# The a and b products of a bilinear layer, taken as seven products of quarters instead of eight

## The chip, the core and the metric

The kernel runs on one core of one Trainium2 chip. The time is that of one execution on the device in microseconds. Before the change it is 843.13 us, the median of 3 runs (842.65 to 844.28). TensorE (PE) multiplies, VectorE (DVE) and ScalarE (ACT) work on tiles in SBUF and in PSUM, GpSimd (POOL) works on SBUF only, and SyncE (SP) issues most transfers.

## The reference, cut to what matters

Attention with decay (4 batches, 8 heads, 576 positions, head size 64) gives x of 2304 tokens by 512. A mixture of 8 experts sends each token through one expert. The last layer takes the result x:

```python
def _moe2_ref(x, w_a, w_b, w_out):
    a = x @ w_a          # 2304x512 @ 512x1536
    b = x @ w_b          # 2304x512 @ 512x1536
    return (a * b @ w_out).astype(np.float32)   # 2304x1536 @ 1536x512
```

All of it is float32.

## The kernel before, in words

Every large product is made of three: an operand v is split into hi, which is v rounded to the fp32r type that PE takes, and lo = v - hi, and PE sums hi*hi, hi*lo and lo*hi in PSUM. So each operand needs a rounding copy and a subtraction somewhere.

The program has three stages on one core: attention with the routing of tokens (to about 127 us), the experts in 8 windows of up to 336 tokens (to 376 us), and the bilinear layer. Each engine has its own instruction list; order comes from semaphores alone. SP, ACT, DVE, POOL and PE each run a loop over pairs of experts, and in the last window of the last expert ACT and DVE also split the first weights of the bilinear layer.

The bilinear layer before the change goes through the tokens in 6 groups of 384 (`GT`). It keeps all of `w_a`, `w_b` and `w_out` split in SBUF, loaded and split once. In a group, for each of 12 feature tiles `f` of 128 features, PE makes a (12 matmuls of 384 columns into `pa`, L1471), then b (12 into `pb`), then the output part of the tile before (`out_part(f - 1)`, 9 matmuls of 512 columns into three `po` banks, L1491). ACT copies a to `a_sb` (L789); DVE multiplies b from PSUM with it (L1138, `g_sb`); ACT rounds the product (L796, `g_hi`); DVE subtracts (L1142, `g_lo`). POOL prepares the tokens of the next group: it rounds `y_in` (L615) and subtracts (L618), 4 tiles of 384 columns each in a group. It also gathers the gates and scatters the finished rows. `pa` and `pb` have two banks each, so DVE and ACT may be a whole feature tile, over 6 us, behind PE.

```python
L1498  for f in range(NF):
L1501      product(0, f, pa[f % 2], a_done)
L1506      product(1, f, pb[f % 2], b_done)
L1507      if f > 0:
L1508          out_part(f - 1)
```

## Time and profile before

| what | us |
|---|---|
| median of 3 runs | 843.13 |
| the profiled execution, whole | 842.02 |
| its span in the profile | 840.3 |
| PE busy, share of the span | 822.5, 98% |
| DVE busy | 325.2, 39% |
| ACT busy | 264.3, 31% |
| POOL busy | 119.7, 14% |
| granted TensorE clock, mean | 0.99 |

The whole execution is 1.7 us longer than its span, which runs from the first instruction of the program to the last. The trace holds one execution. A matmul's time in it goes from its issue to its last result; the next one is issued long before that, so the distance between starts is what a matmul costs. Some matmul records are missing.

### The profile page before, as it was taken

The page shows a single profiled execution, that of the slowest core. Times are in us where ns is not written, and L with a number is a line of the kernel's source. Part 1 is how long each engine was busy: PE and PEld are TensorE (multiplying, and loading weights), DVE is VectorE, ACT ScalarE, POOL GpSimd, SP SyncE. Part 2 cuts the span into 40 slices and gives each one's busy share as a digit, 9 for nine tenths or more (in the row PEclk, how much of TensorE's full clock was granted, in tenths as well). Part 3 has the DMA queues.
Part 4 walks back from the last instruction along what each step waited for, and adds up shares of the span by engine and source line. Part 5 has one row for each costly group of instructions (what it writes and reads, how often), then busy time and mean ns, then how long its engine had stood idle before and what let it go on. Part 6 is the DMA issues. An engine that isn't in the chain of part 4 may idle for free.

```text
span 840.3 us, 14986 instructions
## 1 busy us (share of the span) xinstructions
PE 822.5 (98%) x5561; PEld 768.5 (91%) x5562; DVE 325.2 (39%) x618; ACT 264.3 (31%) x487; POOL 119.7 (14%) x165
## 2 busy tenths in 40 slices
PE   8999989999999999999999999999999999999995
PEld 6888859999999999999999999999999999999994
DVE  5577776464464464473433111211211121121111
ACT  3556634354354354352332111111111111111111
POOL 2000031101101110140503200500140050002001
PEclk9999979999999999999999999999999999999998
DMA  9999827347437438549101100100010010001001
GB/s 190 221 220 232 215 60 245 108 160 266 113 153 265 132 133 265 147 156 315 46 1 38 39 1 0 56 21 1 37 38 0 0 38 0 0 1 38 1 0 39
DMA packets 93144, 83.76 MB, mean 100 GB/s; under 512 B 61085, under 2 KB 73919, under 8 KB 93103
## 3 DMA queue, kind: packets, MB, share of 16 engines
q1 hardware_dynamic: 88591, 71.45, 28.5%
q0 software_dynamic: 4368, 11.71, 4.8%
q8 instruction: 26, 0.43, 0.2%
q14 instruction: 15, 0.12, 0.1%
...
## 4 chain that ended last, share of the span: by engine, by line
PE 96%; DVE 2%; DMA 1%; issue 0%; SPq 0%; ACT 0%; POOLq 0%; POOL 0%; DVEq 0%
PE pa L1471 18%; PE pb L1471 18%; PE po L1491 18%; PE py L1422 14%; PE pu L1411 9%; PE pu L1393 4%; PE pscore L1192 2%; PE pout L1241 2%; PE pu L1401 2%; PE pout L1216 2%; PE px L1370 1%; PE pstate L1228 1%; PE pq L1180 1%; PE px_tok L1203 1%; PE pk L1180 1%; PE pscore L1271 1%
## 5 line engine op out<-in xcount | busy, mean ns | idle before, releaser
L1138 DVE TENSOR_TENSOR g_sb<-pb,a_sb 128x384 f32<-128x384 f32 x72 | 40.2, 558 | 291.3 <-PE pb L1471 291.3
L1471 PE MATMUL pb<-x_hi,w_hi 128*128 128x384 f32 x288 | 97.0, 337 | 0.0
L1471 PE MATMUL pb<-x_lo,w_hi 128*128 128x384 f32 x288 | 97.0, 337 | 0.0
L1471 PE MATMUL pb<-x_hi,w_lo 128*128 128x384 f32 x288 | 96.9, 337 | 0.0
L789 ACT COPY a_sb<-pa 128x384 f32<-128x384 f32 x72 | 34.5, 480 | 195.7 <-PE pa L1471 195.7
L796 ACT CAST g_hi<-g_sb 128x384 fp32r<-128x384 f32 x72 | 36.9, 513 | 162.5 <-DVE g_sb L1138 162.5
L1097 DVE TENSOR_TENSOR w_lo<-land,w_hi 128x1024 fp32r<-128x1024 f32 x64 | 79.7, 1245 | 10.7 <-ACT w_hi L745 10.4
L1422 PE MATMUL py<-h_hi,w_hi 128*128 128x336 f32 x256 | 83.8, 327 | 0.0
L1471 PE MATMUL pa<-x_hi,w_hi 128*128 128x384 f32 x240 | 81.5, 339 | 0.0
L1471 PE MATMUL pa<-x_hi,w_lo 128*128 128x384 f32 x240 | 81.2, 338 | 0.0
L1422 PE MATMUL py<-h_hi,w_lo 128*128 128x336 f32 x256 | 81.1, 317 | 0.0
L1471 PE MATMUL pa<-x_lo,w_hi 128*128 128x384 f32 x240 | 81.0, 337 | 0.0
L1422 PE MATMUL py<-h_lo,w_hi 128*128 128x336 f32 x256 | 80.9, 316 | 0.0
L1491 PE MATMUL po<-w_lo,g_hi 128*128 128x512 f32 x180 | 71.4, 396 | 0.0
L1491 PE MATMUL po<-w_hi,g_lo 128*128 128x512 f32 x180 | 71.1, 395 | 0.0
L1491 PE MATMUL po<-w_hi,g_hi 128*128 128x512 f32 x180 | 71.0, 395 | 0.0
L649 POOL DMA_INDIRECT out_dram<-o_sb,ids_now x18 | 17.8, 989 | 352.9 <-DVE o_sb L1165 281.8
L745 ACT CAST w_hi<-land 128x1024 fp32r<-128x1024 f32 x64 | 66.4, 1048 | 3.8 <-DMA land<-in_moe_w_a_dram 2.8
L1142 DVE TENSOR_TENSOR g_lo<-g_sb,g_hi 128x384 fp32r<-128x384 f32 x72 | 41.4, 574 | 45.0 <-ACT g_hi L796 45.0
L1102 DVE SCALAR_TENSOR_TENSOR h_lo<-pu,h_hi 128x336 fp32r<-128x336 f32 x64 | 32.3, 505 | 57.7 <-ACT h_hi L749 55.9
L1471 PEld LDWEIGHTS pb<-x_hi,w_lo 128*128 128x128 f32 x288 | 54.1, 188 | 0.0
L1471 PEld LDWEIGHTS pb<-x_lo,w_hi 128*128 128x128 f32 x288 | 54.1, 188 | 0.0
...
## 6 DMA issues: line engine op xcount, KB each, us to landing
land<-in_moe_w_dram SPq DMA_DIRECT2D x64, 512.0 KB, 8.7
...
land<-in_moe_w_b_dram SPq DMA_DIRECT2D x6, 512.0 KB, 10.2
```

What stands on the lines that cost most here:

```text
L745: nc.scalar.copy(w_hi[1 - s][:, u, :], land[1 - s][:, u, :]).then_inc(hi_done, 1)
L789: nc.scalar.copy(a_sb[:], pa[f % 2][:, 0:GT]).then_inc(a_kept, 1)
L796: nc.scalar.copy(g_hi[:, f % 2, :], g_sb[:]).then_inc(g_hi_ready, 1)
L1097: nc.vector.tensor_tensor(w_lo[1 - s][:, u, :], land[1 - s][:, u, :], w_hi[1 - s][:, u, :], ALU.subtract).then_inc(lo_done, 1)
L1102: nc.vector.scalar_tensor_tensor(out=h_lo[:, f, :], in0=pu[f % NPU][:, 0:W], scalar=0.0, in1=h_hi[:, f, :], op0=ALU.max, op1=ALU.subtract) ...
L1138: nc.vector.tensor_tensor(g_sb[:], pb[f % 2][:, 0:GT], a_sb[:], ALU.mult).then_inc(prod_done, 1)
L1142: nc.vector.tensor_tensor(g_lo[:, f % 2, :], g_sb[:], g_hi[:, f % 2, :], ALU.subtract).then_inc(g_lo_ready, 1)
L1393: last = nc.tensor.matmul(pu[f][:, 0:W], w[s][:, d, at(f)], x_hi[:, d, :], start=(d == 0 and w is w_hi), stop=False)
L1411: last = nc.tensor.matmul(pu[f % NPU][:, 0:W], w, m[:, d, :], start=(d == 0 and n == 0), stop=(d == DC - 1 and n == 2))
L1422: last = nc.tensor.matmul(py[d][:, 0:W], w, m[:, f, :], start=(f == 0 and n == 0), stop=(f == FF - 1 and n == 2))
L1471: ins = nc.tensor.matmul(acc[:, 0:GT], w[:, cols(d)], x2[:, d, :], start=(d == 0 and n == 0), stop=(d == DC - 1 and n == 2))
L1491: ins = nc.tensor.matmul(po[i][:], m_[:, f % 2, rows], w, start=(f == 0 and n == 0), stop=(f == NF - 1 and n == 2))
```

## The change: what it does

The layer now runs in 3 passes (`pair` in the code) of 768 tokens and, in each, 6 steps of 256 features (`q`): 18 steps (`NIT`). In a step x is seen as four quarters (256 inputs by 384 tokens: B11, B12, B21, B22) and the weights of a, and of b, as four quarters (256 inputs by 128 features: A11 to A22). Winograd's form of Strassen's scheme makes the four result tiles C11, C12, C21, C22 from seven products of sums of quarters. A product is 6 matmuls of 384 columns, so a and b of a step take 2 x 7 x 6 = 84; before, the same work took 96. The output part of a step stays at 36 matmuls of 512 columns and now stands between the seven products of a (kind 0) and of b (kind 1); it is that of the step before.

- Seven products go by turns into two banks `pz0`, `pz1`. A product may begin only when the one two places ahead of it has been read out (`z_kept_act`, `z_kept_dve`). ACT copies the first (`p1`) and, of a, the third (`a_sb`, C11); DVE takes the others, adding `p1`, `u2` or `u3`, 5 in kind 0 and 6 in kind 1. `keep_g11` multiplies C11 of b by a at once; the other three g tiles are finished by `times_a`, g = g * a_sb, both in SBUF.
- The weights of a step (a unit: a or b, 512 KB) are fetched in every pass by 4 transfers (`load_w2`) into one of 3 buffers, combined by DVE (`combine_w2`, 4 operations of 256 columns), rounded by ACT (`high_w2`, 768 and 1024 columns), and their low parts made by POOL (`low_w2`, 768 and 1024 columns). `w_out` is fetched per step (`load_wo`), rounded by ACT, subtracted by DVE (`low_wo`, 1024 columns).
- The tokens of the next pass (`x2`) are combined by POOL (4 operations of 768 columns at q = 1) and made low by POOL (`low_x2`, 768 columns: two at q = 2, 3, 4, one at q = 5). For the first pass DVE combines them in the last expert window (`last_body`) and makes 4 of the 7 low parts.
- Low parts are written over what was fetched. The loops over experts end one pair earlier, and the last two experts and all 18 steps stand written out.

```diff
-    G = 3
-    GT = G * P
-    NG = FT // G
-    NF = F2 // P
+    T = 3 * P
+    NP = N // (2 * T)
+    PT = 2 * T // P
+    NQ = F2 // (2 * P)
+    NIT = NP * NQ
+    DH2 = DC // 2
+    NPR = 7
+    S1, S2, S3, S4, A12, A22, A11, A21 = range(NPR + 1)
+    W_OF = (A11, S2, A12, S3, S1, A22, S4)
+    B11, T2, B21, T3, T1, T4, B22 = range(NPR)
+    FRESH = (0, 1, 4)
+    MADE = (C11, C22, C21, C12)
 ...
+            def load_w2(unit):
+                w = (w_a, w_b)[unit % 2].rearrange("(h j p) (q i f) -> p h q i j f", h=2, j=DH2, p=P, q=NQ, i=2)
+                for half, at in ((0, A11), (1, A12)):
+                    for i in range(2):
+                        sp.dma_start(w2_land[unit % 3][:, at + i, :, :],
+                                     w[:, half, unit // 2 % NQ, i, :, :]).then_inc(w2_in[unit % 3], 16)
 ...
+            def low_w2(unit, part):
+                if part == 0:
+                    pool.wait_ge(w2_made, unit + 1)
+                pool.wait_ge(w2_hi_done, 2 * unit + part + 1)
+                at = slice(A12, A21) if part == 0 else slice(0, A12)
+                nc.gpsimd.tensor_tensor(w2_lo[unit % 3][:, at, :, :], w2_land[unit % 3][:, at, :, :], w2_hi[unit % 3][:, at, :, :],
+                                        ALU.subtract).then_inc(w2_lo_done, 1)
 ...
+            for step in range(NIT):
+                pair, q = step // NQ, step % NQ
+                if step < NIT - 1:
+                    for part in range(2):
+                        low_w2(2 * step + 2, part)
+                if step == 0:
+                    pool.wait_ge(wo_hi_done, 1)
+                    nc.gpsimd.tensor_tensor(wo_lo[0][:], wo_land[0][:], wo_hi[0][:], ALU.subtract).then_inc(wo_lo_pool, 1)
+                if q == 0 and pair > 0:
+                    scatter(pair - 1)
+                if step < NIT - 1:
+                    for part in range(2):
+                        low_w2(2 * step + 3, part)
+                if pair < NP - 1:
+                    if q == 1:
+                        combine_x2(pair + 1)
+                    for k in range(2 * q - 4, min(2 * q - 2, NPR)):
+                        if k >= 0:
+                            low_x2(pair + 1, k)
+                if q == NQ - 1:
+                    gather_gates(pair)
+            scatter(NP - 1)
 ...
+            def high_w2(unit, part):
+                n = unit % 3
+                if part == 0:
+                    act.wait_ge(w2_in[n], 64 * (unit // 3) + 64)
+                    at = slice(A12, A21)
+                else:
+                    act.wait_ge(w2_made, unit + 1)
+                    at = slice(0, A12)
+                nc.scalar.copy(w2_hi[n][:, at, :, :], w2_land[n][:, at, :, :]).then_inc(w2_hi_done, 1)
 ...
+                keep_p1(step, 1)
+                high_w2(2 * step + 3, 0)
+                high_g(step, 0)
+                high_w2(2 * step + 3, 1)
 ...
-            def group(g, par, first, last):
-                for f in range(NF):
-                    dve.wait_ge(b_done, g * NF + (f + 1))
-                    dve.wait_ge(a_kept, g * NF + (f + 1))
-                    if not (first and f == 0):
-                        dve.wait_ge(g_lo_ready, g * NF + f)
-                    nc.vector.tensor_tensor(g_sb[:], pb[f % 2][:, 0:GT], a_sb[:],
-                                            ALU.mult).then_inc(prod_done, 1)
-                    dve.wait_ge(g_hi_ready, g * NF + (f + 1))
-                    nc.vector.tensor_tensor(g_lo[:, f % 2, :], g_sb[:], g_hi[:, f % 2, :],
-                                            ALU.subtract).then_inc(g_lo_ready, 1)
 ...
+            def combine_w2(unit):
+                w = w2_land[unit % 3]
+                dve.wait_ge(w2_in[unit % 3], 64 * (unit // 3) + 64)
+                nc.vector.tensor_tensor(w[:, S3, :, :], w[:, A11, :, :], w[:, A21, :, :], ALU.subtract).then_inc(w2_step, 1)
+                nc.vector.tensor_tensor(w[:, S1, :, :], w[:, A21, :, :], w[:, A22, :, :], ALU.add).then_inc(w2_step, 1)
+                dve.wait_ge(w2_step, 3 * unit + 2)
+                nc.vector.tensor_tensor(w[:, S2, :, :], w[:, S1, :, :], w[:, A11, :, :], ALU.subtract).then_inc(w2_step, 1)
+                dve.wait_ge(w2_step, 3 * unit + 3)
+                nc.vector.tensor_tensor(w[:, S4, :, :], w[:, A12, :, :], w[:, S2, :, :], ALU.subtract).then_inc(w2_made, 1)
 ...
+            def keep_sum(step, kind, k, dst, more, of):
+                n = step_product(step, kind, k)
+                if of == 0:
+                    dve.wait_ge(z_kept_act, kept_by_act(step_product(step, kind, 0)))
+                else:
+                    dve.wait_ge(z_kept_dve, kept_by_dve(step_product(step, kind, of)))
+                dve.wait_ge(multiplied, n + 1)
+                nc.vector.tensor_tensor(dst, pz[n % 2][:, 0:T], more, ALU.add).then_inc(z_kept_dve, 1)
 ...
+            def times_a(step, g, c, k):
+                dve.wait_ge(z_kept_dve, kept_by_dve(step_product(step, 1, k)))
+                nc.vector.tensor_tensor(g[:, c, :], g[:, c, :], a_sb[:, c, :], ALU.mult).then_inc(g_made, 1)
 ...
+                if step > 0:
+                    low_g(step - 1, 0)
+                keep_u2(step, 0)
+                if step > 0:
+                    low_g(step - 1, 1)
+                    low_g(step - 1, 2)
+                keep_u3(step, 0)
+                if step > 0:
+                    low_g(step - 1, 3)
+                keep_c22(step, 0, a_sb)
+                keep_c21(step, 0, a_sb)
 ...
+                    combine_w2(2 * step + 2)
+                    low_wo(step)
 ...
+                keep_u2(step, 1)
+                keep_g11(step, g)
+                keep_u3(step, 1)
+                keep_c22(step, 1, g)
+                times_a(step, g, C22, 4)
+                keep_c21(step, 1, g)
+                times_a(step, g, C21, 5)
+                keep_c12(step, 1, g)
+                times_a(step, g, C12, 6)
 ...
+            def products(step, kind):
+                unit, at = 2 * step + kind, step // NQ % 2
+                for k in range(NPR):
+                    n = step_product(step, kind, k)
+                    if k < 2:
+                        pe.wait_ge(w2_lo_done, 2 * unit + k + 1)
+                    if kind == 0 and step % NQ == 0:
+                        if step > 0:
+                            pe.wait_ge(x2_lo_pool, step // NQ * NPR - 4 + k + 1)
+                        elif k < DC:
+                            pe.wait_ge(x2_lo_dve, k + 1)
+                        else:
+                            pe.wait_ge(x2_lo_pool, k - DC + 1)
+                    if n >= 2:
+                        if (n - 2) % (2 * NPR) in BY_ACT:
+                            pe.wait_ge(z_kept_act, kept_by_act(n - 2))
+                        else:
+                            pe.wait_ge(z_kept_dve, kept_by_dve(n - 2))
+                    for j in range(DH2):
+                        hi, lo = w2_hi[unit % 3][:, W_OF[k], j, :], w2_lo[unit % 3][:, W_OF[k], j, :]
+                        x_hi2, x_lo2 = x2_hi[at][:, k, j, :], x2_lo[at][:, k, j, :]
+                        for i, (w, m) in enumerate(((hi, x_hi2), (hi, x_lo2), (lo, x_hi2))):
+                            ins = nc.tensor.matmul(pz[n % 2][:, 0:T], w, m, start=(k in FRESH and j == 0 and i == 0),
+                                                   stop=(j == DH2 - 1 and i == 2), skip_group_check=True)
+                    ins.then_inc(multiplied, 1)
 ...
+            for step in range(NIT):
+                products(step, 0)
+                if step == 0:
+                    pe.wait_ge(xb_lo, n_windows * DC + DC)
+                    pe.sem_inc(alone_pe, 1)
+                    nc.tensor.transpose(pgate[0:NT, 0:P], gate_t[:].rearrange("p c b -> p (c b)"), ident[:]).then_inc(gates_turned, 1)
+                if step == 1:
+                    pe.wait_ge(ids_in, 16)
+                    pe.wait_ge(gates_turned_out, 1)
+                    nc.tensor.transpose(pgate[:, P:P + FT], id_rows[:], ident[0:FT, 0:FT]).then_inc(ids_turned, 1)
+                if 0 < step < NIT - 1:
+                    out_part(step - 1)
+                products(step, 1)
```

PE around the end of a unit. Before, in the loop over groups: the last matmul of a, then b of the same feature tile (`pa`, `pb` are PSUM banks, `x2` the tokens, `w` the weights).

```order
L1471 MATMUL pa1<-x2_hi1,w_lo1 128x384
L1471 MATMUL pb1<-x2_hi1,w_hi1 128x384 [waits prod_done]
L1471 MATMUL pb1<-x2_lo1,w_hi1 128x384
L1471 MATMUL pb1<-x2_hi1,w_lo1 128x384
L1471 MATMUL pb1<-x2_hi1,w_hi1 128x384
L1471 MATMUL pb1<-x2_lo1,w_hi1 128x384
```

Now, the same engine inside one unit of weights, in a later step (without buffer numbers; `pz` stands for both banks):

```order
L1862 MATMUL pz<-x_hi,w_hi 128x384 [waits z_kept_dve]
L1862 MATMUL pz<-x_lo,w_hi 128x384
L1862 MATMUL pz<-x_hi,w_lo 128x384
L1862 MATMUL pz<-x_hi,w_hi 128x384
L1862 MATMUL pz<-x_lo,w_hi 128x384
L1862 MATMUL pz<-x_hi,w_lo 128x384
L1862 MATMUL pz<-x_hi,w_hi 128x384 [waits z_kept_act]
```

A wait stood every 12 matmuls of 384 columns on something one feature tile old; it stands every 6 now, on the product two places ahead.

DVE at the boundary between two steps. Before, what it does for PE is a pair, L1138 and L1142, once a feature tile; here at the layer's start, where some weights are still split (L1128):

```order
L1138 TENSOR_TENSOR g_sb<-pb0,a_sb 128x384 [waits a_kept,b_done]
L1142 TENSOR_TENSOR g_lo<-g_sb,g_hi 128x384 [waits g_hi_ready]
L1138 TENSOR_TENSOR g_sb<-pb1,a_sb 128x384 [waits g_lo_ready,a_kept,b_done]
L1142 TENSOR_TENSOR g_lo<-g_sb,g_hi 128x384 [waits g_hi_ready]
L1146 COPY gate_rows<-pgate 20x128 [waits gates_turned]
L1128 TENSOR_TENSOR wx_lo<-landx,wx_hi 128x1024 [waits hi_done]
L1138 TENSOR_TENSOR g_sb<-pb0,a_sb 128x384 [waits g_lo_ready,a_kept,b_done]
L1142 TENSOR_TENSOR g_lo<-g_sb,g_hi 128x384 [waits g_hi_ready]
```

Now, from the fifth product of b (L1441 reads PSUM, L1469 is `times_a`, L1475 `low_g`):

```order
L1441 TENSOR_TENSOR g0<-pz1,u3 128x384 [waits multiplied,z_kept_dve]
L1469 TENSOR_TENSOR g0<-g0,a_sb 128x384 [waits z_kept_dve]
L1441 TENSOR_TENSOR g0<-pz0,p1 128x384 [waits multiplied,z_kept_act]
L1469 TENSOR_TENSOR g0<-g0,a_sb 128x384 [waits z_kept_dve]
L1441 TENSOR_TENSOR g0<-pz1,u2 128x384 [waits multiplied,z_kept_dve]
L1469 TENSOR_TENSOR g0<-g0,a_sb 128x384 [waits z_kept_dve]
L1475 TENSOR_TENSOR g_lo0<-g0,g_hi0 128x384 [waits g_hi_ready]
L1441 TENSOR_TENSOR u2<-pz1,p1 128x384 [waits multiplied,z_kept_act]
```

The readouts that free the banks now stand behind operations with both inputs in SBUF.

POOL. Before, the preparation of a group's tokens, four times this pair, once a group:

```order
L615 CAST x2_hi0<-y_in 128x384 [waits y_in_done]
L616 ISA
L618 TENSOR_TENSOR x2_lo0<-y_in,x2_hi0 128x384 [waits x2_step]
L615 CAST x2_hi0<-y_in 128x384
L616 REGISTER_ALU
L618 TENSOR_TENSOR x2_lo0<-y_in,x2_hi0 128x384 [waits x2_step]
```

Now two whole steps of the first pass:

```order
L741 TENSOR_TENSOR w2_lo0<-w2_land0,w2_hi0 128x768 [waits w2_hi_done,w2_made]
L741 TENSOR_TENSOR w2_lo0<-w2_land0,w2_hi0 128x1024 [waits w2_hi_done]
L741 TENSOR_TENSOR w2_lo1<-w2_land1,w2_hi1 128x768 [waits w2_hi_done,w2_made]
L741 TENSOR_TENSOR w2_lo1<-w2_land1,w2_hi1 128x1024 [waits w2_hi_done]
L752 TENSOR_TENSOR x2_lo1<-x2_land1,x2_hi1 128x768 [waits x2_hi_done,x2_made_pool] x2
L741 TENSOR_TENSOR w2_lo2<-w2_land2,w2_hi2 128x768 [waits w2_hi_done,w2_made]
L741 TENSOR_TENSOR w2_lo2<-w2_land2,w2_hi2 128x1024 [waits w2_hi_done]
L741 TENSOR_TENSOR w2_lo0<-w2_land0,w2_hi0 128x768 [waits w2_hi_done,w2_made]
L741 TENSOR_TENSOR w2_lo0<-w2_land0,w2_hi0 128x1024 [waits w2_hi_done]
L752 TENSOR_TENSOR x2_lo1<-x2_land1,x2_hi1 128x768 [waits x2_hi_done,x2_made_pool] x2
```

Eight short operations in 75 us have become four to eight long ones in every step.

## Rows read from the trace of the kernel before

**Rows 1.** Page, busy time by engine: us, share, instructions.
```profile
PE 822.5 (98%) x5561; PEld 768.5 (91%) x5562; DVE 325.2 (39%) x618; ACT 264.3 (31%) x487; POOL 119.7 (14%) x165
```
**Rows 2.** Page, chain that ended last, by engine.
```profile
PE 96%; DVE 2%; DMA 1%; issue 0%; SPq 0%; ACT 0%; POOLq 0%; POOL 0%; DVEq 0%
```
**Rows 3.** Windows: length, then busy PE, PEld, DVE, ACT, POOL, clock, DMA, GB/s.
```profile
345.40:376.25 30.85, 30.85 (x206) 30.66 (x204) 17.61 (x22) 13.87 (x23) 11.87 (x11) 1.00 0.66 206
376.25:451.00 74.75, 74.75 (x395) 69.75 (x394) 27.18 (x38) 21.60 (x35) 11.48 (x12) 1.00 0.32 102
...
831.00:840.30 9.30, 0.00 (x0) 0.00 (x0) 0.85 (x2) 0.00 (x0) 2.94 (x3) 0.64 0.23 85
```
**Rows 4.** Timeline, one feature tile: start, length, engine, line, operation, tiles.
```profile
500.81 0.33 PE L1471 MATMUL pa<-x_hi,w_hi 128*128 128x384 f32 x1
...
502.74 0.33 PE L1471 MATMUL pa<-x_hi,w_lo 128*128 128x384 f32 x1
...
503.11 0.48 ACT L789 COPY a_sb<-pa 128x384 f32<-128x384 f32 x1 [3.01 <-PE pa L1471]
...
504.99 0.39 PE L1491 MATMUL po<-w_hi,g_hi 128*128 128x512 f32 x1
...
507.07 0.33 PE L1471 MATMUL pa<-x_hi,w_hi 128*128 128x384 f32 x1
```
**Rows 5.** Lines by form, 376 to 840: count, busy us, mean ns, idle before.
```profile
L1142 DVE TENSOR_TENSOR g_lo<-g_sb,g_hi 128x384 fp32r<-128x384 f32 x72 | 41.4, 574 | 45.0 <-ACT g_hi L796 45.0
L1138 DVE TENSOR_TENSOR g_sb<-pb,a_sb 128x384 f32<-128x384 f32 x72 | 40.2, 558 | 291.3 <-PE pb L1471 291.3
L796 ACT CAST g_hi<-g_sb 128x384 fp32r<-128x384 f32 x72 | 36.9, 513 | 162.5 <-DVE g_sb L1138 162.5
...
L618 POOL TENSOR_TENSOR x_lo<-y_in,x_hi 128x384 fp32r<-128x384 f32 x20 | 20.8, 1038 | 3.6 <-POOL x_hi L615 3.6
...
L778 ACT CAST w_hi<-land 128x1024 fp32r<-128x1024 f32 x8 | 8.4, 1046 | 0.0
...
L1128 DVE TENSOR_TENSOR wx_lo<-landx,wx_hi 128x1024 fp32r<-128x1024 f32 x2 | 2.4, 1214 | 0.4 <-ACT wx_hi L778 0.4
```
**Rows 6.** Timeline of DVE, then of POOL, 457.9 to 463.5.
```profile
457.93 0.56 DVE L1142 TENSOR_TENSOR g_lo<-g_sb,g_hi 128x384 fp32r<-128x384 f32 x1 [0.58 <-ACT g_hi L796]
...
462.24 0.85 DVE L1142 TENSOR_TENSOR g_lo<-g_sb,g_hi 128x384 fp32r<-128x384 f32 x1 [0.66 <-ACT g_hi L796]
...
461.66 1.01 POOL L618 TENSOR_TENSOR x_lo<-y_in,x_hi 128x384 fp32r<-128x384 f32 x1 [0.19 <-POOL x_hi L615]
462.61 0.83 POOL L615 CAST x_hi<-y_in 128x384 fp32r<-128x384 f32 x1
```
**Rows 7.** Timeline of DVE and of POOL, 466.9 to 468.
```profile
467.37 0.56 DVE L1138 TENSOR_TENSOR g_sb<-pb,a_sb 128x384 f32<-128x384 f32 x1 [4.29 <-PE pb L1471]
...
466.90 1.02 POOL L618 TENSOR_TENSOR x_lo<-y_in,x_hi 128x384 fp32r<-128x384 f32 x1 [0.18 <-POOL x_hi L615]
```
**Rows 8.** Timeline, PE released by DVE, 127 to 129.
```profile
127.36 1.23 DVE L968 TENSOR_TENSOR w_lo<-land,w_hi 128x1024 fp32r<-128x1024 f32 x1
...
128.68 0.42 PE L1393 MATMUL pu<-x_hi,w_hi 128*128 128x336 f32 x1 [0.32 <-DVE w_lo L968]
```
**Rows 9.** Timeline of ACT: last activation of the last expert window.
```profile
361.87 0.44 ACT L749 ACTIVATE h_hi<-pu 128x336 fp32r<-128x336 f32 x1
```
**Rows 10.** DMA issues: count, KB each, median us from issue to landing.
```profile
land<-in_moe_w_b_dram SPq DMA_DIRECT2D x6, 512.0 KB, 10.2
...
landx<-in_moe_w_out_dram SPq DMA_DIRECT2D x1, 512.0 KB, 5.0
```
**Rows 11.** Timeline of POOL: the last scatter of rows.
```profile
833.81 0.96 POOL L649 DMA_INDIRECT out_dram<-o_sb,ids_now  x1 [0.30 <-issue]
```
**Rows 12.** Windows around the routing, columns as in rows 3.
```profile
111.00:117.00 6.00, 3.79 (x56) 2.62 (x54) 5.43 (x31) 1.83 (x6) 3.11 (x5) 0.98 0.13 46
117.00:127.00 10.00, 9.06 (x35) 4.00 (x36) 8.26 (x41) 1.62 (x5) 4.51 (x5) 0.50 0.32 87
```

More of the change, by code:

```diff
@@ new lines, in scatter @@
+            def scatter(pair):
+                at = pair % 2
+                for i in range(PT):
+                    pool.wait_ge(out_kept[i % 2], pair * (PT // 2) + i // 2 + 1)
+                    pool.indirect_dma_start(out, bass.IndirectOffsetOnAxis(ap=ids_now[:, at, i:i + 1].bitcast(u32), axis=0),
+                                            o_sb[i][:], None).then_inc(out_stored, 16)
+            for part in range(2):
+                low_w2(0, part)
+            for k in range(4, NPR):
+                low_x2(0, k)
@@ new lines, in high_wo, with keep_out @@
+            def high_wo(step):
+                act.wait_ge(wo_in[step % 2], 16 * (step // 2) + 16)
+                nc.scalar.copy(wo_hi[step % 2][:], wo_land[step % 2][:]).then_inc(wo_hi_done, 1)
+            def keep_out(pair, i):
+                if i == 0:
+                    act.wait_ge(gates_squared, pair + 1)
+                    if pair == 0:
+                        act.wait_ge(y_stored, n_windows * 16 + 16)
+                    else:
+                        act.wait_ge(out_stored, pair * (16 * PT))
+                act.wait_ge(out_ended, pair * PT + i + 1)
+                nc.scalar.activation(o_sb[i][:], po[i][:], ACT.Copy, scale=gates2[:, pair % 2, i:i + 1]).then_inc(out_kept[0], 1)
@@ new lines, in _ @@
+            for step in range(NIT):
+                pair, q = step // NQ, step % NQ
+                keep_p1(step, 0)
+                if step > 0:
+                    for i in range(1, 4):
+                        high_g(step - 1, i)
+                keep_c11(step)
+                if step == 0:
+                    high_w2(2, 0)
+                    keep_p1(0, 1)
+                    high_w2(2, 1)
+                    high_wo(0)
+                    high_g(0, 0)
+                    continue
+                if step == NIT - 1:
+                    keep_p1(step, 1)
+                    break
+                if step == 1:
+                    high_w2(3, 0)
+                    high_w2(3, 1)
+                high_w2(2 * step + 2, 0)
+                high_w2(2 * step + 2, 1)
+                high_wo(step)
+                if pair < NP - 1:
+                    for k in range(2 * q - 4, min(2 * q - 2, NPR)):
+                        if k >= 0:
+                            high_x2(pair + 1, k)
+                if q == 0:
+                    for i in range(0, PT, 2):
+                        keep_out(pair - 1, i)
+                keep_p1(step, 1)
+                high_w2(2 * step + 3, 0)
+                high_g(step, 0)
+                high_w2(2 * step + 3, 1)
@@ L810, in _ @@
+            high_wo(NIT - 1)
+            for i in range(4):
+                high_g(NIT - 1, i)
+            for i in range(0, PT, 2):
+                keep_out(NP - 1, i)
         @block.vector
@@ new lines, in _ @@
+            for step in range(NIT):
+                pair, q = step // NQ, step % NQ
+                g = g_of(step)[1]
+                if step > 0:
[9 more added lines that the diff above has]
+                keep_c21(step, 0, a_sb)
+                keep_c12(step, 0, a_sb)
+                if step == 0:
+                    combine_w2(2)
+                elif step < NIT - 1:
+                    if step == 1:
@@ L1168, in _ @@
-            groups(dve, group)
+                        combine_w2(3)
+                    combine_w2(2 * step + 2)
+                    low_wo(step)
+                    if q == 0:
+                        square_gates(pair - 1)
+                        keep_out(pair - 1, 1)
+                    combine_w2(2 * step + 3)
+                    if q == 0:
+                        for i in range(3, PT, 2):
+                            keep_out(pair - 1, i)
+                keep_u2(step, 1)
+                keep_g11(step, g)
@@ new lines, in _ @@
+                keep_u3(step, 1)
[5 more added lines that the diff above has]
+                times_a(step, g, C12, 6)
+                if step == 0:
+                    dve.wait_ge(gates_turned, 1)
+                    nc.vector.tensor_copy(gate_rows[:], pgate[0:NT, 0:P]).then_inc(gates_turned_out, 1)
+            low_wo(NIT - 1)
+            for i in range(4):
+                low_g(NIT - 1, i)
@@ L1171, in _ @@
+            square_gates(NP - 1)
+            for i in range(1, PT, 2):
+                keep_out(NP - 1, i)
         @block.tensor
```

548 lines of the change are left out of this document (325 added, 223 removed).

## The prediction

> **What bounds the kernel now.** I read the page's busy shares first: PE is busy 98% of the span [rows 1], and the chain that ended last lies on PE for 96% [rows 2]. The windows by stage then show PE without a hole through the bilinear layer, 376.25 to 831, at a granted clock of 1.00, 2.4 GHz; only the last 9.3 us of the span have no matmul [rows 3]. So a matmul taken away is worth its distance to the next. The timeline of one feature tile gives that: 24 matmuls of 384 columns from 500.81 to 504.99, 0.174 us each; 9 of 512 columns to 507.07, 0.231 each [rows 4]. The other engines have room: DVE has 27 us of work in the first 75 us of the layer and stands idle 291 us in front of `g_sb` [rows 3, 5]. Their slack is what the change spends, so the last views are timelines of DVE beside POOL.
>
> **What goes.** The two products had 6 x 12 x 24 = 1728 matmuls of 384 columns; now there are 18 x 84 = 1512. 216 x 0.174 = 37.6 us. The output part keeps its 648 matmuls. At the end, six row tiles are closed one per 1.4 us instead of three at once, so only the last of the scatters, 0.96 us each and issued 1.3 us apart, comes after PE [rows 11]; that gives about 1.5 us.
>
> **The new pace.** A product is 6 x 0.174 = 1.04 us. A result can be read 0.37 us after its last matmul's start (502.74 to 503.11 [rows 4]), so product k counted from the start of a unit is readable at 1.04k + 1.24. DVE's readout takes 0.56 and ACT's 0.48 [rows 4, 5]. A PE that waits for DVE starts 0.09 us after DVE's end (1.23 us from 127.36, PE at 128.68) and its first matmul is some 0.09 longer, 0.42 against 0.33 [rows 4, 8]: 0.18. So a bank read out at once is free at 1.24 + 0.56 + 0.18 = 1.98, and the product that wants it is due at 2.08. The margin is 0.1 us, where it was a whole feature tile. What can delay a readout is thus the whole question.
>
> **DVE and POOL block each other.** Alone, the subtraction of two SBUF tiles took 0.56 us on DVE. The one that began 0.58 us into POOL's 1.01 us subtraction took 0.85, and ended at 463.09, 0.42 after POOL's end; POOL's next copy, begun at 462.61, ended only at 463.44 [rows 6]. `g_sb`, with one input in PSUM, took its 0.56 in the midst of POOL's operation [rows 7]. I read it so: an operation with both inputs in SBUF stands until POOL's is over, then needs 0.42 more, and the reverse.
>
> The Trainium skill (SBUF — State Buffer, "Who interferes with whom") states this as an exclusive lock on a shared port: DVE with two SBUF inputs against a POOL operation that reads SBUF, held for the whole instruction. The trace agrees for POOL operations of 1.0 us; longer ones it doesn't show. By the page the delay grows with POOL's operation, which is my forecast; if it were bounded at what the rows show, it would be the first rival.
>
> POOL's new operations are long. 384 columns take 1.01 to 1.04 [rows 5, 6], so at the same rate 768 take 2.0 and 1024 take 2.7. A step has two of each, 9.4 us, and up to 4 x 2.0 for the next pass's tokens. DVE has 8 two-input operations of 256 columns (0.42), 7 of 384 (0.56) and one of 1024 (1.21), 8.5 us. A step of PE is 84 x 0.174 + 36 x 0.231 = 22.9 us. The two engines exclude each other for 17.9 to 26 of it.
>
> **One boundary between steps, from the start of b's products.** g11 (product 2) is readable at 3.3, DVE has it by 3.9, ACT's `high_g` runs to 4.5 (0.51) and `high_w2` part 1 to 5.55 (1.05 for 1024 columns [rows 5]). POOL starts `low_w2` part 1 at 5.65 and ends at 8.34. DVE reads c22 (product 4) from 5.40 to 5.96 and asks for `times_a` at 6.04: it stands until 8.34 and ends at 8.76. Behind it is the readout of c21, 8.76 to 9.32. PE's next product wants that bank and was due at 7.29; it starts at 9.5. **2.2 us of wait at each of the 17 boundaries: 37 us.**
>
> If POOL also has `low_x2`, that is granted at 8.76 and ends at 10.64; the second `times_a` ends at 11.06, c12 is read by 11.62, and the next product starts at 11.8 instead of 10.5: 1.3. The second `low_x2` ends at 12.95 and the third `times_a` at 13.4; u2 of the new step is read by 14.4, 0.7 too late for its product 3. **2.0 more at the 10 boundaries after q = 1 to 5 of the first two passes: 20 us**, and after q = 1, with four combining operations, about 2.3 more each, 4.5.
>
> **The rest of a step.** During the output part (8.3 us) DVE does two `combine_w2` (1.8 each) and `low_wo`, POOL two `low_w2`, 4.7: with the exclusions 11 us of work in a row, and u2 of b is due 10.6 after a's last product. DVE's keeps of a take little room; I cost it at nothing, with up to 1 us a step if it slips. The transfers: 512 KB landed in 5.0 us for the first of a train and 10.2 in the midst of one [rows 10]. A unit comes alone now, in four pieces; I take 6, nearer to the lone one. `high_g`, `high_wo` and the token copies on ACT lie under the output part.
>
> **The start.** ACT ends the last activation of the last window at 361.87 + 0.44, 13.9 us before PE's first product at 376.25 [rows 3, 9]. In that time DVE has 4 + 4 two-input operations of 768 columns (0.98 each by the rate of the rows for 384 and 1024), 4 of 256, 1.7, and POOL two `low_w2` (4.7) and three `low_x2` (6.1): 20.3 us that exclude each other, and DVE's 4 window readouts (about 2) besides. So unit 1 is combined some 6 us after PE begins. ACT's rounding of it (1.05) and its two copies of y (0.9) stand in its queue ahead of `p1`, which product 2 waits for, due at 2.1 and free near 8.5: 6.4. The y store and so unit 2's fetch are late by the same, and `p1` of b stands behind the rounding of unit 2: 3 more. With the repair of this in step 1, 15 us; bounds 5 and 22.
>
> **Sum.** 842.0 (the profiled execution) - 37.6 - 1.5 + 37 + 20 + 4.5 + 15 = 879.4; the median of before is 1.1 above its profiled execution, so 880.
>
> **Unknown costs.** The rate of POOL on long operations: with 10% less, each block shortens by 0.27, some 9 us over all; with a tenth more, 9 longer. Fetching the weights in every pass: between nothing and 1.4 us at 16 steps, 22 us, if every unit lands after 10.2 us. The clock: after a stretch with PE busy 3.8 of 6 us the clock was granted at half for 10 us, 1.2 GHz [rows 12]. PE will be busy some 85% of a step, so I expect full clock there; the long wait at the start may cost one such stretch, up to 5 us. Longer written-out code: nothing, as the first and last group before were written out too and ran without a hole; 5 us at most.
>
> **The rivals.**
> - *The block is short.* The rows show no delay above 0.5 us on either side. If an operation of 2.7 us doesn't hold the other out for its length, `times_a` is 0.4 late, and a boundary costs about 1.0: 17, and at the start 8. 842.0 + 1.1 - 37.6 - 1.5 + 25 = 829; with nothing lost at all it would be 804. The change breaks even where the waits of PE come to 38 us, 2.1 a step; this lies below. For it: no operation as long as 2.7 us was ever seen to hold DVE out. Against: in the row that began 0.58 in, DVE waited for just what was left of POOL's operation.
> - *Only the first collision counts.* If POOL's part 1 comes once a step and `low_x2` falls beside the readouts, 37 + 8 of waits remain: 842.0 + 1.1 - 37.6 - 1.5 + 45 = 849. For it: order within a microsecond decides. Against: POOL runs its operations back to back, so the next one always stands ready when DVE ends.
> - *The transfers are late too.* Four pieces of 128 KB a unit, in short rows, land after 10.2 us instead of 6; combining slips past u2 of b by 1.4 us in 16 steps. 880 + 22 = 902. Against: SP's queue holds one unit at a time.
>
> **Chances.** Forecast 0.65 (863 to 896); short block 0.12; first collision only 0.12; late transfers 0.11. Range 846 to 904: it leaves out the short block and the tails, about 0.2. What this kernel's measurement can tell from no change is 0.2%, 1.7 us. Faster is the short block and a sliver of the second rival, 0.13; same 0.01; slower 0.86.
>
> **What would show it.** In the profile after: PE's distance between matmuls of 384 columns still 0.174 at clock 1.00; PE idle near 75 us in the layer, released by DVE's readouts of the seventh and sixth product (L1441), some 2.2 us ahead of a step's first product; `times_a` (L1469) with a mean far above 0.56; POOL's L741 at 2.0 and 2.7; the steps of the third pass shorter by some 2 us than those of the first two; a wait of about 6 us on ACT's `p1` right after the last expert. The prediction is wrong if L1469 stays near 0.56, or if PE's waits lie on `w2_lo_done`, that is on POOL and the transfers.

## The result

The changed kernel takes 880.13 us (median of 4 runs, 879.14 to 881.12) against 842.89 for the kernel before (842.12 to 844.28): a ratio of 1.044, interval 1.0421 to 1.0458. It is slower by 37 us, where 38 were forecast. The sum came out right, but in part by luck: its terms for PE's waits were too large, another, the clock, was missing from it, and the two nearly cancel.

The page of the profile after (profiled run 880.36 us, span 878.2): busy time, the granted clock over the span in 40 slices, and the chain that ended last.

```profile
PE 808.1 (92%) x5345; PEld 745.8 (85%) x5346; DVE 573.0 (65%) x944; ACT 330.3 (38%) x565; POOL 284.6 (32%) x211
...
PEclk9999969999999999989999999989999999999999
...
PE 78%; DVE 11%; issue 8%; ACT 2%; POOL 1%; another core or an unknown queue 0%; POOLq 0%; DVEq 0%; ACTq 0%
```

PE has 216 matmuls fewer than in [rows 1] and the span is longer; the chain, 96% on PE in [rows 2], is now 78% on PE. The groups of lines (count, busy us, mean ns, idle before and its releaser) and the DMA issues say where to look:

```profile
L1862 PE MATMUL pz<-x_hi,w_hi 128*128 128x384 f32 x504 | 181.0, 359 | 53.3 <-DVE g L1441 38.4
...
L1469 DVE TENSOR_TENSOR g<-g,a_sb 128x384 f32<-128x384 f32 x54 | 83.3, 1542 | 1.9
...
L1441 DVE TENSOR_TENSOR u<-pz,p 128x384 f32<-128x384 f32 x72 | 40.1, 557 | 58.0 <-PE pz L1862 54.7
L1480 DVE TENSOR_TENSOR wo_lo<-wo_land,wo_hi 128x1024 fp32r<-128x1024 f32 x17 | 54.1, 3182 | 33.1 <-ACT wo_hi L1012 33.1
...
w_land<-in_moe_w_a_dram SPq DMA_DIRECT2D x72, 128.0 KB, 2.3
```

L1469, `times_a`, does the same work as L1142 in [rows 5], one subtraction or product of 384 columns in SBUF, and takes 1542 ns instead of 574. L1441, with one input in PSUM, stayed at 557. PE's idle time is put down to L1441, the readout of `g`: it is only the instruction behind `times_a` in DVE's queue. L1480, `low_wo`, is held longest of all, 3182 ns against 1214 for 1024 columns in [rows 5]; it runs during the output part, and no wait of PE is put down to it. The weights land in 2.3 us, and no wait of PE is put down to their transfers.

One boundary between two steps, in the timelines of DVE, POOL and PE (start, length, ..., idle before and releaser):

```profile
483.15 0.56 DVE L1441 TENSOR_TENSOR g<-pz,u 128x384 f32<-128x384 f32 x1 [0.48 <-PE pz L1862]
483.74 2.24 DVE L1469 TENSOR_TENSOR g<-g,a_sb 128x384 f32<-128x384 f32 x1
485.90 0.55 DVE L1441 TENSOR_TENSOR g<-pz,p 128x384 f32<-128x384 f32 x1
486.48 1.60 DVE L1469 TENSOR_TENSOR g<-g,a_sb 128x384 f32<-128x384 f32 x1
488.00 0.55 DVE L1441 TENSOR_TENSOR g<-pz,u 128x384 f32<-128x384 f32 x1
...
483.18 2.39 POOL L741 TENSOR_TENSOR w_lo<-w_land,w_hi 128x1024 fp32r<-128x1024 f32 x1 [1.08 <-ACT w_hi L948]
485.52 4.24 POOL L752 TENSOR_TENSOR x_lo<-x_land,x_hi 128x768 fp32r<-128x768 f32 x2
...
486.60 0.41 PE L1862 MATMUL pz<-x_hi,w_hi 128*128 128x384 f32 x1 [1.45 <-DVE g L1441]
...
488.70 0.41 PE L1862 MATMUL pz<-x_hi,w_hi 128*128 128x384 f32 x1 [0.81 <-DVE g L1441]
...
489.43 0.52 PE L1862 MATMUL pz<-x_hi,w_hi 128*128 128x384 f32 x1
489.75 0.52 PE L1862 MATMUL pz<-x_lo,w_hi 128*128 128x384 f32 x1
```

POOL's subtraction ends at 483.18 + 2.39 = 485.57. `times_a`, asked for at 483.74, ends at 485.98, 0.41 later; the second one ends 0.44 after the first `low_x2` (485.52 + 2.12 = 487.64). This is the lock of [rows 6], with POOL operations twice as long. PE waits twice, and from 489.43 its matmuls lie 0.32 us apart instead of 0.174: the clock has fallen. Windows of a quiet stretch, of one with the boundary, and of what came behind it (length, busy PE, PEld, DVE, ACT, POOL, clock, DMA, GB/s):

```profile
468.00:482.00 14.00, 14.00 (x71) 12.59 (x70) 8.80 (x14) 5.06 (x7) 5.97 (x3) 1.00 0.24 75
482.00:496.00 14.00, 11.74 (x57) 11.16 (x57) 11.22 (x15) 4.13 (x8) 6.68 (x4) 0.88 0.14 39
...
489.10:492.50 3.40, 3.40 (x13) 3.40 (x12) 3.04 (x5) 0.64 (x2) 0.67 (x1) 0.50 0.00 0
```

The chain of waits through the same boundary shows how such a lock looks in that view:

```profile
483.74 0.41 DVE g L1469
484.15 1.75 issue
485.90 0.56 DVE g L1441
```

The time in which DVE stood behind POOL is called "issue", time in which it waited for nothing that the profile shows. No row names POOL. Of the 66 us of "issue" in the chain (8%, before 0%) 50 stand like this between a `times_a` and the readout behind it.

At a change of passes the wait is longer. DVE, POOL and PE:

```profile
566.11 5.07 DVE L1469 TENSOR_TENSOR g<-g,a_sb 128x384 f32<-128x384 f32 x1
...
565.65 0.96 POOL L788 DMA_INDIRECT out_dram<-o_sb,ids_now  x1 [0.30 <-issue]
566.64 4.12 POOL L741 TENSOR_TENSOR w_lo<-w_land,w_hi 128x768 fp32r<-128x768 f32 x2
...
571.80 0.66 PE L1862 MATMUL pz<-x_hi,w_hi 128*128 128x384 f32 x1 [4.30 <-DVE g L1441]
```

Six scatters of finished rows, one per 1.3 us, held back POOL's first low part; both low parts then ran back to back, and one `times_a` waited for the two. The second change of passes looks the same: `times_a` from 735.37 takes 4.91 us.

The start of the layer, DVE, POOL, ACT and PE:

```profile
376.07 2.09 DVE L1384 TENSOR_TENSOR w_land<-w_land 128x256 f32<-128x256 f32 x1
377.84 3.97 POOL L752 TENSOR_TENSOR x_lo<-x_land,x_hi 128x768 fp32r<-128x768 f32 x2
378.08 2.07 DVE L1385 TENSOR_TENSOR w_land<-w_land 128x256 f32<-128x256 f32 x1
...
382.58 1.04 ACT L948 CAST w_hi<-w_land 128x1024 fp32r<-128x1024 f32 x1 [4.90 <-DVE w_land L1389]
...
384.83 0.66 PE L1862 MATMUL pz<-x_hi,w_hi 128*128 128x384 f32 x1 [4.76 <-ACT p L992]
```

Sums of 256 columns, 0.42 us alone, took 2.1 beside POOL's; unit 1 was combined at 382.55, 4.7 after PE's first product at 377.84 (6 forecast).

**The balance**, from the distances between the starts of PE's matmuls, from the first of the layer (377.8) to the last (870.3), each less 0.174 or 0.231. Where the distance was over 0.3 us too long, 36 places, 59 us in all: 15 ordinary boundaries of 1.6 = 24.4, two changes of passes of 4.4 = 8.8, ten second waits of 0.97 = 9.7, the start 8.9, three waits behind the combining of tokens 4.3, three others 3.1 (1.9 of it at 560.43, on ACT's `p`, which stands behind ACT's copies of finished rows). The layer is 492.5 us long, and 412.4 with no loss (run 1 below, less its own waits), so 80.1 are lost. The other 21 are the clock: it was granted at half, 1.2 GHz, in 11 stretches of 44 us in all, and the distances in them that are not among the 36 are 19.5 us too long together.

### The profile page after: what moved, and what is told of

Read it like the earlier page. It is cut to its first block, busy times and chain, and to the rows that moved or that the text cites. A ratio compares the mean times of both kernels' runs of the same rounds, so it can differ in the third digit from the quotient of the medians.

```text
span 878.2 us, 14879 instructions
## 1 busy us (share of the span) xinstructions
PE 808.1 (92%) x5345; PEld 745.8 (85%) x5346; DVE 573.0 (65%) x944; ACT 330.3 (38%) x565; POOL 284.6 (32%) x211
## 4 chain that ended last, share of the span: by engine, by line
PE 78%; DVE 11%; issue 8%; ACT 2%; POOL 1%; another core or an unknown queue 0%; POOLq 0%; DVEq 0%; ACTq 0%
PE pz L1862 25%; PE po L1889 14%; PE py L1805 12%; PE pu L1794 9%; PE pu L1776 3%; DVE g L1441 3%; PE pscore L1575 2%; PE pout L1624 2%; PE pu L1784 2%; PE pout L1599 2%; DVE g L1469 1%; PE pq L1563 1%; PE px_tok L1586 1%; PE pstate L1611 1%; PE px L1753 1%
## 5 line engine op out<-in xcount | busy, mean ns | idle before, releaser
L741 POOL TENSOR_TENSOR w_lo<-w_land,w_hi 128x768 fp32r<-128x768 f32 x72 | 153.1, 2139 | 238.9 <-DVE w_land L1389 156.6
L1862 PE MATMUL pz<-x_hi,w_hi 128*128 128x384 f32 x504 | 181.0, 359 | 53.3 <-DVE g L1441 38.4
L1862 PE MATMUL pz<-x_hi,w_lo 128*128 128x384 f32 x504 | 177.2, 352 | 0.0
L1862 PE MATMUL pz<-x_lo,w_hi 128*128 128x384 f32 x504 | 177.2, 352 | 0.0
L1862 PEld LDWEIGHTS pz<-x_hi,w_hi 128*128 128x128 f32 x504 | 100.9, 200 | 66.0 <-POOL w_lo L741 31.9
L1862 PEld LDWEIGHTS pz<-x_lo,w_hi 128*128 128x128 f32 x504 | 100.8, 200 | 0.6
L1862 PEld LDWEIGHTS pz<-x_hi,w_lo 128*128 128x128 f32 x504 | 100.7, 200 | 0.0
L1469 DVE TENSOR_TENSOR g<-g,a_sb 128x384 f32<-128x384 f32 x54 | 83.3, 1542 | 1.9
L1889 PE MATMUL po<-wo_hi,g_hi 128*128 128x512 f32 x216 | 84.2, 390 | 0.0
L1889 PE MATMUL po<-wo_hi,g_lo 128*128 128x512 f32 x216 | 84.2, 390 | 0.0
L1889 PE MATMUL po<-wo_lo,g_hi 128*128 128x512 f32 x216 | 84.2, 390 | 0.0
L1441 DVE TENSOR_TENSOR u<-pz,p 128x384 f32<-128x384 f32 x72 | 40.1, 557 | 58.0 <-PE pz L1862 54.7
L1480 DVE TENSOR_TENSOR wo_lo<-wo_land,wo_hi 128x1024 fp32r<-128x1024 f32 x17 | 54.1, 3182 | 33.1 <-ACT wo_hi L1012 33.1
L1360 DVE SCALAR_TENSOR_TENSOR h_lo<-pu,h_hi 128x336 fp32r<-128x336 f32 x56 | 28.3, 505 | 50.4 <-ACT h_hi L917 48.9
```

Source lines behind the costliest of these rows:

```text
L741: nc.gpsimd.tensor_tensor(w2_lo[unit % 3][:, at, :, :], w2_land[unit % 3][:, at, :, :], w2_hi[unit % 3][:, at, :, :], ALU.subtract).then_i ...
L1360: nc.vector.scalar_tensor_tensor(out=h_lo[:, f, :], in0=pu[f % NPU][:, 0:W], scalar=0.0, in1=h_hi[:, f, :], op0=ALU.max, op1=ALU.subtract) ...
L1441: nc.vector.tensor_tensor(dst, pz[n % 2][:, 0:T], more, ALU.add).then_inc(z_kept_dve, 1)
L1469: nc.vector.tensor_tensor(g[:, c, :], g[:, c, :], a_sb[:, c, :], ALU.mult).then_inc(g_made, 1)
L1480: nc.vector.tensor_tensor(wo_lo[step % 2][:], wo_land[step % 2][:], wo_hi[step % 2][:], ALU.subtract).then_inc(wo_lo_dve, 1)
L1862: ins = nc.tensor.matmul(pz[n % 2][:, 0:T], w, m, start=(k in FRESH and j == 0 and i == 0), stop=(j == DH2 - 1 and i == 2), skip_group_che ...
```

## The experiments

Each kernel starts from the changed one. The code cuts leave out the semaphore updates (`.then_inc`); in pieces, the last piece of an operation makes the update. The kernel before took 842.45 us beside the first four runs and 842.60 beside the last three.

**1. POOL's preparations only write.** Left out are the low parts made on POOL and the sums of the tokens for passes 2 and 3: zeros are written in their place.

```diff
-nc.gpsimd.tensor_tensor(w2_lo[..][:, at, :, :], w2_land[..][:, at, :, :], w2_hi[..][:, at, :, :], ALU.subtract)
+nc.gpsimd.memset(w2_lo[..][:, at, :, :].bitcast(f32), 0.0)
 ... (x2_lo and the four sums of x2 likewise)
```

> All of POOL's preparations (low parts of the weights and of the tokens, sums of the tokens of passes 2 and 3) are replaced by writes of zero over as many columns, so POOL reads no SBUF there; the low parts are left out of the result. Theory (DVE with two SBUF inputs and a POOL operation that reads SBUF exclude each other for the whole instruction): times_a falls from a mean of 1.54 us to 0.56, PE's waits at the step boundaries go, and with them the stretches at half clock. 842.9 - 37.6 - 1.5 + 5 to 10 for the start: 812 us, 806 to 822. Rival A (DVE alone is too slow for the readouts, POOL does not matter): 878 to 882, times_a unchanged. Rival B (each block is bounded by some 0.5 us): cannot be, or the gain is 20 us at most, 860.

Measured: 800.59 us (800.33 to 801.14), ratio to before 0.9502, interval 0.9486 to 0.9518. Lines of DVE and POOL, then the window of the layer:

```profile
L1465 DVE TENSOR_TENSOR g<-g,a_sb 128x384 f32<-128x384 f32 x54 | 30.8, 570 | 1.9
...
L741 POOL MEMSET w_lo<- 128x1024 f32 x35 | 33.4, 955 | 36.9 <-ACT w_hi L944 36.9
```
```profile
376.30:790.30 414.00, 412.85 (x2164) 382.77 (x2162) 250.92 (x492) 152.76 (x238) 111.83 (x130) 1.00 0.28 86
```

POOL writes beside DVE for 0.96 us at a time and `times_a` stays at 570 ns; 28 of the 54 ran while POOL wrote, each in 0.56 or 0.57 us. POOL operations that read no SBUF tile held nobody. DVE has the same 944 instructions as in the changed kernel, so it was not too slow by itself. PE is busy 412.85 of 414.0 us at full clock. This is the reference for what follows: with POOL's SBUF-to-SBUF work 78.5 us went from the layer, those of the start and the clock included; 1.6 us of waits are left. The run came 11 us below the 812 expected, and below the range (806 to 822): the start, put at 5 to 10, costs next to nothing (PE's first product at 376.30 against 376.25 before, 1.3 us of waits behind it), and the layer lost 4 us more than the matmuls that I had counted.

**2. Only the work for the next passes' tokens writes.** The low parts and sums of x2 for passes 2 and 3 are left out; `low_w2` stays.

```diff
 def low_x2(pair, k):
+    if pair == 0:
         nc.gpsimd.tensor_tensor(x2_lo[at][:, k, :, :], ...)
+    else:
+        nc.gpsimd.memset(x2_lo[at][:, k, :, :].bitcast(f32), 0.0)
 ... (the four sums of x2 also by memset)
```

> Only POOL's work on the tokens of passes 2 and 3 is replaced by writes of zero; the weights' low parts stay. Theory: the first wait of about 1.65 us stays at all boundaries, the second (about 1.0) goes, and the steps of passes 1 and 2 get as long as those of pass 3 (24.5 us instead of 27.1): 10 x 2.6 and about 8 for the two boundaries after the sums: 846 us, 840 to 852. Rival A: 880.

Measured: 851.49 us (849.73 to 851.85), ratio 1.0099, interval 1.0079 to 1.0119. PE's waits of this kernel:

```profile
PE pz L1863 <- DVE g L1442: 28.3, 16, 4.2
PE pz L1863 <- ACT p L993: 4.7, 1, 4.7
PE pz L1863 <- DVE u L1442: 3.8, 2, 3.4
```

The wait of 1.6 us stands at every ordinary boundary as before; the ten second waits are gone, and the one in front of `g` is now 28.3 us over 16 times, against 38.4 over 27. The run is 28.6 us faster than the changed kernel, and 5 above the 846 expected, in the range. In the profiled executions the layer is 29.4 us shorter, of which the waits make up 18. The other 11 are the clock: 4 stretches at half, 20 us, instead of 11 and 44. They follow the waits of 4.9, 3.6, 4.4 and 3.8 us; no boundary with a single wait of 1.6 us has one.

**3. POOL's operations in pieces** of 256 columns (weights) and 384 (tokens), the same columns in all. Nothing is left out.

```diff
-ins = nc.gpsimd.tensor_tensor(w2_lo[..][:, at, :, :], w2_land[..][:, at, :, :], w2_hi[..][:, at, :, :], ALU.subtract)
+for t in range(at.start, at.stop):
+    ins = nc.gpsimd.tensor_tensor(w2_lo[..][:, t, :, :], w2_land[..][:, t, :, :], w2_hi[..][:, t, :, :], ALU.subtract)
 ... (x2_lo and the sums of x2: for j in range(DH2))
```

> POOL's same work in pieces of 256 columns (weights) and 384 columns (tokens), nothing left out. Theory: a block lasts at most what is left of a piece, 0.6 to 1.0 us, since DVE gets its turn between two pieces: waits of PE shrink by some 30 us and the half clock by some 10: 840 us, 828 to 856. If the exclusion were kept over back-to-back POOL operations, or if the total of POOL's busy time counted: 878 or more.

Measured: 826.10 us (825.38 to 826.57), ratio 0.9799, interval 0.9783 to 0.9816. Lines of POOL and DVE:

```profile
L743 POOL TENSOR_TENSOR w_lo<-w_land,w_hi 128x256 fp32r<-128x256 f32 x252 | 221.1, 910 | 118.5 <-DVE w_land L1396 74.0
...
L1482 DVE TENSOR_TENSOR g_lo<-g,g_hi 128x384 fp32r<-128x384 f32 x72 | 66.9, 951 | 0.0
L1476 DVE TENSOR_TENSOR g<-g,a_sb 128x384 f32<-128x384 f32 x54 | 33.6, 622 | 1.9
```

The same bytes, and POOL is busy longer (362 us against 285), yet the kernel is 54 us faster. So it is not the traffic but the length of one POOL instruction that DVE waits for. `times_a` fell from 1542 to 622 ns; `g_lo`, which stands further back in the step, rose from 610 to 951, as POOL's work now ends later. Gaps above 0.3 us sum to 20, and one stretch at half clock is left. The time is 14 us below the 840 expected, 2 below the range: I had kept blocks of 0.6 to 1.0 us, and PE's waits at ordinary boundaries are 0.3 to 0.4.

**4. The 1024-column low part on DVE** from unit 3 on; POOL keeps the rest whole.

```diff
+def low_made(unit):
+    dve.wait_ge(w2_hi_done, 2 * unit + 2)
+    nc.vector.tensor_tensor(w2_lo[unit % 3][:, 0:A12, :, :], w2_land[..][:, 0:A12, :, :], w2_hi[..][:, 0:A12, :, :], ALU.subtract)
 ... (called for each unit from 3 on; POOL's loop drops that part, and each part has its own semaphore)
```

> From the fourth unit on DVE makes the low part of the four sums (1024 columns, 1.2 us) that POOL made in 2.4 us, during the output part. Nothing left out. Theory: the operation that starts just before times_a is gone; the token work of POOL in passes 1 and 2 still collides: 840 us, 828 to 856, and the steps of pass 3 without any wait. Rival A (DVE is overloaded): it has 2.4 us more in each step, so slower than 880.

Measured: 831.17 us (830.61 to 832.80), ratio 0.9868, interval 0.9849 to 0.9887.

```profile
L1468 DVE TENSOR_TENSOR g<-g,a_sb 128x384 f32<-128x384 f32 x54 | 48.2, 892 | 1.9
```

33 more operations of 1.2 us on DVE, and the kernel gains 49 us (840 were expected, 828 to 856): DVE was not short of time, it stood behind POOL; its busy time even fell, from 573 to 538 us. What is left at most boundaries of the first two passes is 1.0 us behind `low_x2`.

**5. Only the weights' low parts in pieces**, the tokens' whole: the edit of 3 at L741 alone.

> Only the subtractions of w2_lo on POOL (line 741) go in pieces of 256 columns; those of x2_lo and the sums of x2 stay whole instructions of 768 columns, as in the changed kernel (880.1 us). The run with all of POOL's work in pieces took 826.1, the run with x2's work as writes 851.5. 
Measured: 844.18 us (839.97 to 845.25, 10 runs), ratio 1.0011, interval 0.9998 to 1.0024. DVE, POOL and PE behind a boundary, and the window there:

```profile
480.60 3.82 DVE L1477 TENSOR_TENSOR g_lo<-g,g_hi 128x384 fp32r<-128x384 f32 x2
484.35 0.54 DVE L1443 TENSOR_TENSOR u<-pz,p 128x384 f32<-128x384 f32 x1
...
479.74 4.26 POOL L754 TENSOR_TENSOR x_lo<-x_land,x_hi 128x768 fp32r<-128x768 f32 x2
...
484.94 0.45 PE L1864 MATMUL pz<-x_hi,w_hi 128*128 128x384 f32 x1 [1.80 <-DVE u L1443]
```
```profile
482.00:488.00 6.00, 4.20 (x23) 3.75 (x22) 4.98 (x8) 0.75 (x1) 2.00 (x1) 1.00 0.00 0
```

The time is 4 us above the 840 expected, in the range, but it did not come about in the way I gave. The waits behind `times_a` are gone, the second one too, which I had kept. In pieces, the weights' work ends later, and the two whole `low_x2` now fall on `g_lo` (mean 1105 ns) instead of `times_a`: one wait of 1.95 at each of those boundaries. The collision moved to the next operation with both inputs in SBUF. (The expectation speaks of a shared input bank; no run shows a bank, only that both operations read SBUF.) The clock came back in the main: 1.00 right behind such a wait, and 17 us at half in the layer instead of 44. The distances in these stretches are 7.0 us too long instead of 19.5, so 12.5 us are won where 18 were forecast. Of six single waits of 1.95 only one, at 509.9, is followed by a stretch at half.

**6. Both 3 and 4.**

> Both earlier edits together: POOL's remaining work in pieces of 256 and 384 columns, and the 1024-column half of w2_lo on DVE from unit 3 on. Theory: each removes what the other leaves (in pieces alone 826.1 us, 20 us of gaps above 0.3 us in the layer; DVE's part alone 831.2, with gaps of 25.7). POOL then has some 270 columns less to do beside each boundary, so the boundary waits go, and what stays is the layer's start, about 12 us, and the slower DVE at two points: 813, range 806 to 822. Rival, that DVE is now the bound at the boundaries, since it does 17 x 2 more instructions of 1.2 us ahead of the readouts: 826 or more, with PE waiting for g or g_lo at every boundary.

Measured: 820.79 us (818.97 to 822.69), ratio 0.9743, interval 0.9720 to 0.9765. Faster than either, 8 us above the forecast but within its range. Boundary waits are 0.4 us.

**7. As 6, and the start reordered.**

```diff
 def last_body(b):                                   # ACT
     high_w2(1, 0)
-    high_w2(1, 1)                                   # now in step 0, behind keep_c11
 ...
-    combine_w2(1)                                   # DVE: now behind the y copies
```

> The kernel of the run before this one in the list, and beside it the start of the layer put in another order: ACT makes the 1024-column high part of unit 1 only after its first two readouts of pz instead of ahead of the last y copies, and DVE copies y_out ahead of the second combination of weights. Theory: the wait of 4.9 us at the layer's start (PE for ACT's p) goes, some 4 us in all, and nothing else moves: 809, range 802 to 818, and 3 to 6 us below the run before it. Rival, that PE is held at the start by the high part itself, which now comes later: no gain, or a loss of up to 3 us.

Measured: 819.72 us (818.76 to 819.88), ratio 0.9723, interval 0.9707 to 0.9740: 1 us below run 6, which their spread hardly tells apart, not the 4 expected, and above the range (802 to 818). PE and a window of run 6, then of run 7:

```profile
382.23 0.42 PE L1881 MATMUL pz<-x_hi,w_hi 128*128 128x384 f32 x1 [2.99 <-ACT p L998]
391.63 0.44 PE L1881 MATMUL pz<-x_hi,w_hi 128*128 128x384 f32 x1 [1.71 <-ACT p L998]
```
```profile
381.00:392.00 11.00, 8.06 (x45) 7.57 (x46) 4.35 (x10) 2.78 (x7) 5.63 (x8) 1.00 0.89 214
```
```profile
381.87 0.62 PE L1881 MATMUL pz<-x_hi,w_hi 128*128 128x384 f32 x1 [2.22 <-DVE u L1447]
```
```profile
381.00:392.00 11.00, 10.13 (x50) 10.02 (x51) 5.59 (x12) 4.23 (x5) 6.69 (x10) 0.84 0.78 189
```

Both waits for `p` are gone, 5.0 us with what they cost around them. In their place stands one of 2.4, since DVE's readout waits behind `combine_w2` in DVE's own queue, and behind it one stretch of 3.4 us at half clock, which costs about 1.6: 5.0 - 2.4 - 1.6 = 1.0. The two profiled executions differ by 0.3.

## Why the prediction was right, and where its terms were not

**What goes: too small by 4.** With nothing in the way the layer takes 412.4 us (414.0 in run 1, less its 1.6 of waits) against 454.3 before, 41.9 less and not 37.6. In the kernel before, distances longer by less than 0.3 us each had added 4.2 us; I had multiplied matmuls by 0.174 and left these out. The tail gave 1.8 (7.9 us from the last matmul to the end of the span, 9.7 before); 1.5 were forecast.

**DVE and POOL block each other: right, the step on which all rested.** Traced at 2.4 us (485.98 against 485.57) and shown by runs 1, 3 and 4, which take away the reading, the length and the instruction. The Trainium skill (SBUF — State Buffer, "SBUF: two separate sides") has the lock held for the whole instruction by the one that starts first. On the length the trace agrees, with 1542 ns in the mean and 0.41 us from POOL's end to DVE's. On the order it does not always: `times_a` at 566.11 and 735.37 began 0.53 and 0.36 us ahead of POOL's subtraction and was the one held. The rival of the short block (829) is refuted.

**The first wait, 2.2 us at 17 boundaries: too large.** It is 1.6 at 15 of them. I took POOL's rate from 384 columns, 2.6 ns each; 1024 columns took 2.39 us in the boundary shown, 2.33 ns a column. POOL also began earlier against `times_a` (0.56 ahead of it, 0.39 forecast), so it ended at 485.57 where the timetable had it 0.5 later. PE's handover cost more than the 0.18 written: 0.15 from DVE's end (486.45) to PE's start and 0.08 on the first matmul, 0.41 against 0.33. At two boundaries the wait was 4.4, by the scatters, which I had not put in POOL's queue. Together 33 where 37 were written.

**The second and third collision, 2.0 at 10 boundaries: twice too large.** The second wait is 0.97 (1.3 forecast). The third `times_a` is held at eight of the ten; after q = 5, with one `low_x2`, it is not (0.56 us at 541.71 and 710.64). The wait of 0.7 that I put behind it came once, at full clock, and as 0.3:

```profile
517.82 0.34 PE L1862 MATMUL pz<-x_hi,w_lo 128*128 128x384 f32 x1
518.29 0.44 PE L1862 MATMUL pz<-x_hi,w_hi 128*128 128x384 f32 x1
```

At five boundaries PE was at half clock by then, so the product needed the bank later than DVE was done with it (491.26 against 492.3 in the boundary shown). At the two after q = 1 it is among the waits behind the combining of tokens, which cost 4.3 (4.5). The second wait alone makes 9.7 instead of 20.

**The start, 15: measured 10.5**, 1.6 on the first product and 8.9 of waits, on `p` and then on `u`.

**The clock, the step that failed.** I wrote "I expect full clock there", since PE would be busy some 85% of a step, and gave it 5 us at most, outside the sum. It took 21. I had judged a step by its mean, while the waits come as a pair: 1.6 and 0.97 us within 2.1 us, and behind six of the ten such pairs matmuls run 0.32 us apart for 3.4 us; the other five stretches follow the waits at the start, at the two changes of passes and just ahead of one. The third pass, with the first wait alone, has no such stretch:

```profile
790.49 0.41 PE L1862 MATMUL pz<-x_hi,w_hi 128*128 128x384 f32 x1 [1.51 <-DVE g L1441]
814.99 0.41 PE L1862 MATMUL pz<-x_hi,w_hi 128*128 128x384 f32 x1 [1.44 <-DVE g L1441]
```

Its steps take 24.5 us. In the first two passes it is 27.1 with such a stretch and 26.0 without (513.71 to 539.72). I forecast a difference of 2, and would have taken 2.6 for a match of the waits; the second wait is 1.0 of it, the clock most of the rest. Runs 2 and 5 part the two causes: without the second wait no ordinary boundary has a stretch, and of six single waits of 1.95 us one has.

**The sum with measured sizes:** 842.0 - 41.9 - 1.8 + 33.2 + 9.7 + 4.3 + 10.5 + 3.1 + 21 = 880.1, against 880.4 in the profiled run. The forecast had 76.5 of waits, where 60.8 were measured, and 39.1 for what goes, where 43.7 went: 20.3 us too much in all. The missing clock made up for it. That the total was met within 1 us is luck; the lock, which carries most of the waits, is not. The "only the first collision" case (849) is what run 2 made on purpose: 851. Late transfers are refuted by landings of 2.3 us.

**What stays open:** why two POOL operations in a row pass ahead of one DVE operation at both changes of passes (566.11, 735.37), where at 483.74 and 486.48 DVE was let in between. POOL was ending a scatter when these two began; a gather on POOL (541.53 to 542.52) didn't hold the `times_a` at 541.71. And how the clock is decided: four of the ten pairs and five of the six single waits of 1.95 us did not lower it.
